# A hand-written beginning for all engines of a delta-rule attention kernel: two tiles' keys in other PSUM banks, the first pair's block inverses on VectorE, zeroing stores issued later

## The reference

```python
k_n = k / (np.linalg.norm(k, axis=-1, keepdims=True) + 1e-06)
for t in range(S):
    kt, vt, bt = (k_n[:, :, t], v[:, :, t], beta[:, :, t, None])
    y[:, :, t] = np.einsum('bhd,bhde->bhe', q[:, :, t], state)
    v_old = np.einsum('bhde,bhd->bhe', state, kt)
    state = state + bt[:, :, :, None] * np.einsum('bhd,bhe->bhde', kt, vt - v_old)
...
    logits = x @ w_gate + modality_bias[modality_id]
    e_idx = np.argmax(logits, axis=1)
...
        h = np.maximum(x[mask] @ w1[e], 0.0)
        out[mask] = gate_w[mask, None] * (h @ w2[e])
...
    h = np.maximum(np.maximum(x @ w1, x @ w2), x @ w3)
    return (h @ w_out).astype(np.float32)
```

## Time and profile before

| | |
|---|---|
| median of 3 runs | 1029.39 us (1027.04 to 1036.47) |
| the profiled execution | 1028.81 us, of which the span is 1027.0 us |
| TensorE (PE) busy | 899.1 us, 88% of the span |
| VectorE (DVE) busy | 668.5 us, 65% |
| ScalarE (ACT) busy | 485.2 us, 47% |
| GpSimd (POOL) busy | 274.6 us, 27% |
| granted TensorE clock, mean | 0.972 |

### The profile page before, as it was taken

The page is one execution under the profiler, slowest core; times in us unless marked ns, Lnnn a source line. Parts: engine busy times, 40 slices in busy tenths (PEclk is TensorE's granted clock), DMA queues, the critical chain, the costliest instruction groups (busy, mean ns, idle before and its releaser), DMA issues.

```text
span 1027.0 us, 29203 instructions
## 1 busy us (share of the span) xinstructions
PE 899.1 (88%) x10418; PEld 668.3 (65%) x10418; DVE 668.5 (65%) x1628; ACT 485.2 (47%) x1080; POOL 274.6 (27%) x677
## 2 busy tenths in 40 slices
PE   3338889999899889559899998999999999999998
PEld 2228878888788878448777776777645454555544
DVE  5336887988798878678987977976752433333231
ACT  3223556666576655446836737545533232323212
POOL 2644455785768672310000000001101010100000
PEclk9997998999999999869999999999999999999999
DMA  6466575556434441068527547387502020101000
GB/s 163 78 175 167 127 188 124 133 148 134 106 77 116 75 105 59 32 217 303 198 94 239 211 135 246 116 249 281 173 1 63 1 62 1 62 17 44 15 16 31
DMA packets 214806, 122.69 MB, mean 119 GB/s; under 512 B 161649, under 2 KB 199537, under 8 KB 214673
## 3 DMA queue, kind: packets, MB, share of 16 engines
q1 hardware_dynamic: 136368, 68.41, 23.2%
q10 hardware_dynamic: 75232, 43.07, 15.5%
q0 software_dynamic: 3072, 9.44, 2.9%
HBM read 69.63 MB, written 26.87 MB: 94 GB/s over the span
## 4 chain that ended last, share of the span: by engine, by line
PE 42%; POOL 15%; DVE 12%; issue 9%; DMA 8%; SPq 8%; DVEq 3%; ACT 2%; ACTq 0%; POOLq 0%
PE psum L1666 20%; PE psum L1685 7%; PE psum L1601 5%; POOL arena L720 5%; POOL arena L717 4%; DMA arena<-blocks 4%; SPq L650 4%; PE psum L1614 4%; SPq L631 3%; DVE arena L1248 3%; DMA arena<-arena 3%; DVE arena L1167 2%; DVE arena L1238 2%; DVE arena L1260 1%; DVEq L1253 1%
## 5 line engine op out<-in xcount | busy, mean ns | idle before, releaser
L1666 PE MATMUL psum<-arena 128*128 128x512 f16 x972 | 212.4, 379 | 0.4 <-DVE arena L1311 0.4
L1666 PEld LDWEIGHTS psum<-arena 128*128 128x128 f16 x972 | 95.0, 98 | 112.5 <-DVE arena L1311 0.8
L1601 PE MATMUL psum<-arena 128*128 128x128 f16 x2232 | 148.3, 222 | 13.1 <-DMA arena<-arena 5.6
L1601 PEld LDWEIGHTS psum<-arena 128*128 128x128 f16 x2232 | 134.8, 99 | 32.8 <-issue 9.2
L1614 PE MATMUL psum<-arena 128*128 x744 | 143.5, 330 | 4.1 <-DVE arena L1238 3.8
L779 POOL DMA_INDIRECT arena<-y_sorted,arena x24 | 22.7, 946 | 462.0 <-PE psum L1601 288.6
L1359 DVE SCALAR_TENSOR_TENSOR arena<-psum,arena 128x512 f32<-128x512 f32 x36 | 27.0, 750 | 141.7 <-PE psum L1666 141.7
L846 ACT ACTIVATE arena<-psum 128x256 f16<-128x256 f32 x144 | 52.1, 379 | 94.9 <-PE psum L1446 94.3
L1614 PEld LDWEIGHTS psum<-arena 128*128 128x128 f16 x744 | 69.0, 99 | 38.0 <-issue 7.6
L972 ACT ACTIVATE arena<-psum 128x256 f16<-128x256 f32 x124 | 47.2, 380 | 94.4 <-PE psum L1601 94.2
L1167 DVE SCALAR_TENSOR_TENSOR arena<-arena 128x384 f16<-128x384 f32 x128 | 74.1, 620 | 5.9 <-ACT arena L803 3.3
(11 more groups left out here) (232 smaller groups left out, 1804.8 us busy)
## 6 DMA issues: line engine op xcount, KB each, us to landing
arena<-arena SPq DMA_DIRECT2D x62, 384.0 KB, 3.6
arena<-in_moe_w_dram ACTq DMA_DIRECT2D x57, 384.0 KB, 4.1
arena<-inverses SPq DMA_DIRECT2D x24, 512.0 KB, 5.2
arena<-in_moe_w_dram SPq DMA_DIRECT2D x16, 384.0 KB, 4.5
y_sorted<-arena ACTq DMA_DIRECT2D x31, 192.0 KB, 3.6
x_sorted<-arena SPq DMA_DIRECT2D x7, 768.0 KB, 6.3
arena<-in_k_dram SPq DMA_DIRECT2D x24, 192.0 KB, 3.4
arena<-in_v_dram ACTq DMA_DIRECT2D x24, 192.0 KB, 3.3
```

The costliest lines, as they stand in the source:

```text
L1601: last = nc.tensor.matmul(psum[:, n % 2, fc * P:fc * P + P], w1[:, at:at + P], xT16[:, s, y, kc * P:kc * P + P], start=(i == 0), stop=(i = ...
L1666: last = nc.tensor.matmul(psum[:, 2 + 3 * (f % 2) + m, :], up_weight(w, m, kc, f), x16[:, par, kc, x, :], start=(i == 0), stop=(i == len(t ...
```

## The change

`run_attention` first runs a list `BEGIN` for each engine, written out by hand, and then goes through the slots as before and leaves out what `BEGIN` has done. `BEGIN` takes the keys of tiles 0 to 5 through `K` before the first merge on TensorE. Tiles 1 and 3 (`OTHER_BANKS`) have their transposed keys and products in banks EB = 4, 5, which nothing else uses until the first `E`. The first pair is eliminated by VectorE (`first inverses`), the other pairs by GpSimd as before. On SP, `block in` of pair 1 stands ahead of `inv out` of pair 0, the small loads (`wgate`, `biasm`, `modid`) and the two zeroing stores into `inverses` follow `k` of tile 4 and not those of tiles 3 and 2. The start of the routing stands behind `K` of tile 4.

```diff
+        BEGIN = {
+            "PE": [("Tk", 0), ("Tk", 1), ("KK", 0), ("KK", 1), ("Tk", 2), ("KK", 2), ("Tk", 3), ("KK", 3),
+                   ("Tk", 4), ("KK", 4), ("Tk", 5), ("KK", 5)],
+            "ACT": [("square", 0), ("root", 0), ("square", 1), ("root", 1), ("square", 2), ("Tk", 0), ("root", 2),
+                    ("square", 3), ("Tk", 1), ("square", 4), ("N0", 0), ("N1", 0), ("Tk", 2), ("root", 3), ("root", 4),
+                    ("N0", 1), ("N1", 1), ("square", 5), ("Tk", 3), ("root", 5), ("N0", 2), ("N1", 2), ("square", 6),
+                    ("Tk", 4), ("N0", 3), ("N1", 3), ("N0", 4), ("N1", 4), ("root", 6), ("Tk", 5)],
+            "DVE": [("sum", 0), ("sum", 1), ("norm", 0), ("sum", 2), ("norm", 1), ("norm", 2), ("K1", 0), ("K0", 0),
+                    ("K1", 1), ("K0", 1), ("sum", 3), ("norm", 3), ("sum", 4), ("K1", 2), ("K0", 2), ("norm", 4), ("sum", 5),
+                    ("K1", 3), ("K0", 3), ("norm", 5), ("first inverses", 0), ("K1", 4), ("K0", 4), ("start routing", 0),
+                    ("sum", 6), ("norm", 6), ("K1", 5), ("K0", 5)],
+            "POOL": [("kn", 0), ("kn", 1), ("kn", 2), ("N0", 0), ("N1", 0), ("kn", 3), ("N0", 1), ("N1", 1), ("kn", 4),
+                     ("N0", 2), ("N1", 2), ("kn", 5), ("N0", 3), ("N1", 3), ("F1", 3), ("F2", 3), ("kn", 6)],
+            "SP": [("k", 0), ("k", 1), ("k", 2), ("k", 3), ("k", 4), ("k", 5), ("k", 6), ("block out", 0), ("block out", 1),
+                   ("block in", 1), ("block out", 2), ("k", 7), ("block out", 3), ("k", 8), ("block in", 3), ("w", 4), ("w", 5),
+                   ("inv out", 0), ("inv in", 0), ("inv in", 1), ("block out", 4), ("k", 9), ("inv out", 2), ("inv in", 2),
+                   ("inv in", 3), ("block out", 5), ("block in", 5)],
+        }
+        OTHER_BANKS = (1, 3)
...
+            for what, t in BEGIN[engine]:
+                step(what, t)
             for slot in range(-10, NT + 12):
                 for what, ahead in ORDER[engine]:
                     t = slot + ahead
+                    if (what, t) in BEGIN[engine]:
+                        continue
...
+        def key_banks(t):
+            return EB if t in OTHER_BANKS else FB
...
+        def eliminate(engine, ops, pair, rows_of):
+            g = nb[:, pair % 2]
+            for m in rows_of:
+                n = SB - 1 - m
+                made = ft[:, 0:m * n].rearrange("p (a b) -> p a b", a=m)
+                at = 28 * pair + 2 * (m - 1)
+                need(engine, solve, at)
+                ops.tensor_tensor(made, g[:, 0:m, m:m + 1].to_broadcast([P, m, n]),
+                                  g[:, m:m + 1, m + 1:SB].to_broadcast([P, m, n]), ALU.mult).then_inc(solve, 1)
+                engine.wait_ge(solve, at + 1)
+                ops.tensor_tensor(g[:, 0:m, m + 1:SB], g[:, 0:m, m + 1:SB], made, ALU.add).then_inc(solve, 1)
...
-                if what == "F1" and t % 2 == 1:
+                if what == "F1" and t % 2 == 1 and pair > 0:
...
+                if what == "first inverses":
+                    dve.wait_ge(block_in[0], 16)
+                    dve.wait_ge(const_ok, 6)
+                    eliminate(dve, nc.vector, 0, range(1, 15))
+                    both_inverses(dve, nc.vector, 0)
...
                 if what == "Tk":
                     pe.wait_ge(kn_ok, t + 1)
-                    need(pe, na_ok[0], begun["KK"])
-                    need(pe, qk_ok[0], begun["KQ"])
+                    need(pe, na_ok[0], keys_in[key_banks(t)])
+                    if key_banks(t) == FB:
+                        need(pe, qk_ok[0], begun["KQ"])
```

More of the change, by code:

```diff
@@ L609, in step @@
                     sp.dma_start(kraw[:, t % KR], source(k, t)).then_inc(k_in[t % KR], 16)
[L610 to L615 removed]
+                    if t == 4:
                         sp.dma_start(wgate[:, :, :], w_gate.rearrange("(c p) e -> p c e", p=P)).then_inc(small_in, 16)
@@ L621, in step @@
                                          modality_id.bitcast(i32).rearrange("(b c p w) -> b p c w", b=B, p=P, w=2)[b]).then_inc(small_in, 16)
+                        sp.wait_ge(zero_ok, 2)
+                        for i in range(2):
+                            sp.dma_start(inverses[i].rearrange("p a h x c -> p a (h x c)"),
+                                         zeros.unsqueeze(1).to_broadcast([P, 2, 2 * H * P])).then_inc(clear_in, 16)
                 if what == "block out":
@@ L737, in step @@
                                             ALU.subtract).then_inc(nlo_ok[g], 1)
-                if what == "F1" and t % 2 == 1:
+                if what == "F1" and t % 2 == 1 and pair > 0:
                     pool.wait_ge(block_in[pair % 2], 16 * (pair // 2 + 1))
-                    eliminate(t, range(1, 8))
-                if what == "F2" and t % 2 == 1:
-                    eliminate(t, range(8, 15))
-                    pool.wait_ge(solve, 28 * (pair + 1))
-                    if pair >= 2:
-                        pool.wait_ge(inv_out[pair % 2], P // SB * 16 * (pair // 2))
-                    g = nb[:, pair % 2]
-                    nc.gpsimd.tensor_tensor(fo[:, pair % 2, 0], g.rearrange("p r c -> p c r"), eye3, ALU.add).then_inc(fo_ok, 1)
-                    nc.gpsimd.tensor_tensor(fo[:, pair % 2, 1], g, eye3, ALU.add).then_inc(fo_ok, 1)
+                    eliminate(pool, nc.gpsimd, pair, range(1, 8))
+                if what == "F2" and t % 2 == 1 and pair > 0:
+                    eliminate(pool, nc.gpsimd, pair, range(8, 15))
+                    both_inverses(pool, nc.gpsimd, pair)
                 if what == "R":
@@ L1056, in step @@
                     nc.vector.tensor_reduce(nrm[:, t % 2, 0, :], square[:, :, :], axis=AX.X, op=ALU.add).then_inc(ss_ok, 1)
-                    if t == 4:
-                        start_routing()
+                if what == "first inverses":
[3 more added lines that the diff above has]
+                    both_inverses(dve, nc.vector, 0)
+                if what == "start routing":
+                    start_routing()
                 if what == "norm":
@@ L1419, in step @@
                             kh = kT[HP * g:HP * g + HP, t % KD, r, :]
-                            last = nc.tensor.matmul(cols(bank(FB[g]))[:, r, :], kh, kh, start=True, stop=True)
+                            last = nc.tensor.matmul(cols(bank(key_banks(t)[g]))[:, r, :], kh, kh, start=True, stop=True)
                             if r == PAIRS - 1:
@@ L1564, in counted @@
                     begun[what] += 1
+                if what == "Tk":
+                    turned_in[key_banks(t)] = t + 1
+                if what == "KK":
+                    keys_in[key_banks(t)] = t + 1
             run_attention("PE", counted)
```

58 lines of the change are left out of this document (26 added, 32 removed).

## The result

The changed kernel takes 1018.94 us in the median of five runs (1012.03 to 1020.28), the kernel before 1030.86 in five runs beside it (1027.04 to 1036.47). The ratio is 0.9891 with a 95% interval of 0.9863 to 0.992: 1.1% faster, 11 us, where 18 were forecast. The median lies inside the range given, 8 us above the forecast. The profiled execution took 1012.03 us, with a span of 1010.2. It is the fastest of the five; the other four took 1018.06 to 1020.28.

What follows compares the result with a forecast made beforehand. The beginning was taken as bound by the chain eliminate, store inverses, store blocks, read blocks (30.2 us a pair). Starting pair 2's elimination 18.2 us sooner gave 1028.8 - 18.2 = 1010.6, with 0.6 for the median 1011 us; range 1005 to 1019.5.

Steps and rivals of the forecast that it cites:

- the zeroing stores at nothing: Beginning, SyncE's queue: moving the 2 MB zeroing stores into `inverses` was costed at nothing.
- the other estimate: Read of 512 KB of inverses: 2.0 us plus bytes at 436 GB/s gives 3.2 us, forecast 2.0 us lower.
- the sum is 18.2 us: Whole attention: pair 2's elimination starts at 75.0 instead of 93.20, and this lead reaches the end, 1028.8 to 1010.6.
- VectorE has no other work due there: Before pair 0's elimination: `K` of tile 3 done by about 29.7, so VectorE is free when blocks arrive at 30.7.
- 28 x 0.23 = 6.5: Pair 0's elimination on VectorE: 28 dependent operations take 6.5 us, 7.4 with two closing ones; 3.8 us gained over GpSimd.
- 21.6 us: TensorE, first merge to `S` of tile 0: 21.6 us instead of 26.5, ends 20.1 and 23.3, `S` at 73.2.
- the forecast's 75.0: End of `kn` of tile 7, when pair 2 can be eliminated: 75.0 us, 1.8 us after `S` starts.
- the median of the runs lies 0.6 above that execution: Whole kernel: 0.6 us added to the profiled execution's 1010.6 to forecast the median, 1011 us.
- The lead shrinks to TensorE's start: Rival: TensorE sets the pace after the start, only the first merge's 10.9 us count, 1017.9 us; chance 0.20.
- The leading loop: Rival: TensorE catches up with the 21 us pair 1 gains and runs at full clock, 1006.8 us; chance 0.10.
- the case of nothing: Rival: something unmoved at the attention's end holds the experts back, 1029 us; chance 0.06.
- The later queue: Rival: a burst after pair 2's read slows the loop by 2 to 4 us a pair, up to 1051 us; chance 0.04.

Runs made afterwards that it cites:

- Experiment 5: Changed kernel with ScalarE's square of tile 4 moved behind the copy of tile 2's keys and the root of tile 3; 1014.67 us, ratio 0.9841.
- Experiments 4: Changed kernel with GpSimd's `N0`, `N1` of tile 3 held back until VectorE has eliminated the first pair; 1007.31 us, ratio 0.9801.
- Experiment 6: Changed kernel with tile 4's square later on ScalarE and VectorE's first elimination ahead of tile 5's norm; 1011.73 us, ratio 0.98.
- experiment 7: Experiment 6 with weight loads and `x_sorted` zeroing of slots 6 and 7 issued ahead of the inverses' store; 1012.3 us, ratio 0.9824.
- the second profiles: Both kernels run and profiled once more, unchanged, in a separate series; before 1026.49 us, changed 1011.55 us.
- experiment 10: The changed kernel once more, unchanged, beside the kernel before on the same chip; 1011.55 us, ratio 0.9848.

## Why the prediction was off in size

**Right.** The sign; the two parts of the change and their order on the queues; pair 0's read at 27.17 (27.2 forecast); the cost of a small operation on VectorE (0.13 to 0.22, forecast 0.20); the store, landing and read of the inverses (42.94 to 55.81, 12.9 us, forecast 13.3); pair 1's elimination on GpSimd, closed by 53.7 (52.4); pair 2 released by `S` of tile 0; the zeroing stores at nothing; the read of the inverses at 5.2 us (5.1 measured, the median of 24, not the 3.2 of the other estimate). After `kn` of tile 7 the pace was the old one.

**What failed** is the size of "the sum is 18.2 us": the mechanism held, and four of its terms were off, in the order of time. **The first** is "VectorE has no other work due there: `K` of tile 3 is done by about 29.7". It was done at 32.0, and with the `norm` behind it the elimination started 2.4 us after the 30.7 at which the forecast had the blocks. I had followed VectorE's and SyncE's lists but not ScalarE's, where a square with one buffer held back tile 2's copy. Experiment 5 mends it alone: 30.18.

**The second** is the term "28 x 0.23 = 6.5", 7.4 with the closing. It measured 9.7. The bounds, 6.4 and 11.8, held it, but for another reason: not larger operations, three blocked ones. The rows of VectorE that I priced from the earlier trace rows stood at times when GpSimd had nothing to do. The twin of the one on 192 elements, 1 us later in the same trace, stood beside an operation of GpSimd and took 1.32 us instead of 0.36:

```profile
26.85 1.32 DVE L1203 TENSOR_TENSOR arena<-arena 128x192 f32<-128x192 f32 x1
```

```profile
26.80 1.16 POOL L736 TENSOR_TENSOR arena<-arena 128x512 f16<-128x512 f32 x1 [3.20 <-ACT arena L840]
```

So the trace of the kernel before had the price in it. Experiments 4 and 6 bring the elimination to 8.1 and 7.9.

**The third**, "21.6 us" from the first merge to `S`, is 22.4: 0.8 more, inside its ends of 20.1 and 23.3. The term took TensorE's rate as given, and it isn't: with the change the products came at the faster rate (experiment 7 shows both) only 15.8 us after the first merge (at 71.6), in the kernel before 7.0 us after it, and in experiment 7, with 6.1, the whole stretch took 19.2. Blocks landed a little faster than the 3.5 us I took: in experiment 6 the elimination starts 2.2 us after the read's issue. Together 2.4 + 2.3 + 0.8, less 0.5 in the inverses' way, are 5.0 us, which is the forecast's 75.0 against `kn`'s end at 79.95.

**The fourth** is how "the sum is 18.2 us" was taken. It counts from 93.20, where pair 2's elimination started before. But its keys were ready at 90.78, and for 2.4 us it waited for its blocks, a wait inside the loop that I credited as lasting gain. The lead to carry forward was 90.78 - 75.0 = 15.8. Such waits come back: in the changed kernel pair 3's elimination waits 4.95 us for its blocks, where it had waited 1.85 (it starts 12.2 us sooner, 112.02 against 124.25). In the second profiles the waits are 6.75 and 3.82. The changed kernel's first:

```profile
112.02 0.21 POOL L542 TENSOR_TENSOR arena<-arena 128x14 f32<-128x14 f32 x1 [4.95 <-DMA arena<-blocks]
```

Experiment 6 meets the forecast's beginning. Its pair 2 starts 18.5 us sooner (74.72), its last elimination closes 16.6 sooner (354.7) and its experts start 14.3 sooner. So the forecast's lead of 18.2 was reached there and not kept. How much of the loss is this wait and how much the difference between two profiles isn't separated.

So the attention's 18.2 become 15.8 by the fourth step, 10.8 by the first three, and 9.5 at the experts' start. The measured 11.2 (by the ratio) and 15.6 in experiment 10 (1.52% of 1026.6) both lie above that. In experiment 10's series the two profiles are 15.3 us apart at the experts' start (457.36 and 442.04).

**Luck, and one more term.** The forecast for the profiled execution was 1010.6, and it took 1012.03. That is no hit: 9.5 us came from the attention, 7.2 from behind it. And "the median of the runs lies 0.6 above that execution" was read off the kernel before. With the change the median lies 6.9 above the profiled execution, and by the number this alone is most of the 8 us by which 1011 was missed. Why the profiled execution was the fastest by 6 us isn't known.

**The rivals.** "The lead shrinks to TensorE's start", 1017.9, is nearest to the median by its number, and wrong as a mechanism. Against the first profile of the kernel before, the first merge with the change is 6.7 us sooner, yet 9.5 arrive; in experiment 6 it is 11.1, and 14.3 arrive. The leading loop and the case of nothing didn't happen. The later queue did show after pair 2: tile 6's eight stores take 6.70 us to issue where eight took 3.7, but the loop did not stay slow.

**Open.** Why the attention before took 7.6 us more in one profile than in the other. The lower granted clock goes with it, and no run separates the two. For the same reason it stays open why the gain measured 11 us in one series and 16 in another: there is no profile of the runs that weren't profiled. That the slow operations wait for GpSimd rests on their ends and on moving GpSimd's work in experiments 4 to 6, not on the same work with other operands.

## What to carry to other kernels

When work moves to an idle engine, read what its neighbour engines do at that very time, and follow the written order of every engine that feeds it, not only of the two that change: a wait for a single buffer on a third engine cost as much as the faster engine gained. Carry forward the lead of the last event that nothing but the moved chain releases, and leave out waits that the steady loop will bring back. Compare the marks inside the trace across variants, and take a second profile of each side: the early marks (first merge, one `kn`) differed by at most 1.5 us between two profiles of one kernel, and so separate 3 us where medians of 1020 us hardly do. The start of the next phase differed by 7.6.

## What the runs showed of the hardware

Short operations of VectorE with two operands in on-chip memory, on 26 or 36 elements a partition, took 0.70, 1.07 and 1.08 us instead of 0.2 while GpSimd ran operations of two operands on 384 or 512 elements, and the two whose neighbour's end is seen ended 0.04 us after it. It met norms of 8 elements too:

```profile
22.23 2.26 POOL L772 TENSOR_TENSOR arena<-arena 128x512 f16<-128x512 f32 x2 [6.69 <-ACT arena L871]
```

```profile
23.61 0.90 DVE L1102 SCALAR_TENSOR_TENSOR arena<-arena 128x8 f32<-128x8 f32 x1
24.55 0.17 DVE L1104 SCALAR_TENSOR_TENSOR arena<-arena 128x8 f32<-128x8 f32 x1
```

The first of the two ends at 24.51, GpSimd's pair at 24.49. It goes the other way too: GpSimd's first operation of pair 1's elimination took 0.50 us at 42.06, beside VectorE's closing one of pair 0, and the same operation of pair 2 took 0.22 at 79.91. Beside VectorE's `K` (42.78 to 44.93), which reads one operand from the accumulators, GpSimd's operations from 43.01 on kept their 0.23 to 0.27.

The Trainium skill names this: "GPSIMD Engine Reference", section "Specifications", says that GpSimd shares its interfaces to on-chip memory with VectorE and contends with VectorE's instructions that take two such operands. The trace agrees, and shows the size: the short one ended when the long one did. I had left it out of the forecast, because the elimination left GpSimd.
